# Channel-major filter and U for the first transform, with separate places for x

## What is computed

```python
h_filt = (np.maximum(pos_emb @ w1, 0) @ w2) * np.exp(-0.01 * pos)[:, None]   # 12480 x 128
u = x * v                                                                    # 12480 x 128
y = irfft(rfft(u, n=2*S) * rfft(h_filt, n=2*S))[:S]                          # per channel
a = x * y
a = np.maximum(a @ w_in, 0)**2 @ w_out                                       # 128 -> 2048 -> 128
h = a @ w_in2
out = (h / (1 + np.exp(-1.702 * h))) @ w_out2
```

## Time and profile before

| | |
|---|---|
| median of three runs | 1559.16 us |
| profiled execution | 1559.6 us |
| its span, first to last instruction | 1557.8 us |
| PE busy | 98% of the span |
| granted TensorE clock, mean | 0.998 |
| filter stage | 0 to 62.5 us |
| first transform, first half and second half | 62.5 to 117.5 and 246 to 299 us |
| inverse of the first half | 166.6 to 243 us |
| perceptrons | from 430 us |

### The profile page before, as it was taken

The page is one execution under the profiler, slowest core; times in us unless marked ns, Lnnn a source line. Parts: engine busy times, 40 slices in busy tenths (PEclk is TensorE's granted clock), DMA queues, the critical chain, the costliest instruction groups (busy, mean ns, idle before and its releaser), DMA issues.

```text
span 1557.8 us, 22645 instructions
## 1 busy us (share of the span) xinstructions
PE 1532.8 (98%) x7860; PEld 1458.2 (94%) x7860; DVE 992.7 (64%) x1315; ACT 943.0 (61%) x1217; POOL 270.0 (17%) x313
## 2 busy tenths in 40 slices
PE   7999999999989999999999999999999999999998
PEld 5898889988779999999999999999999999999997
DVE  4867686676656666666666666666666666666664
ACT  3353003431067777777777777777777777777775
POOL 5706791177710000000000000000000000000000
PEclk9999999999999999999999999999999999999999
DMA  7454720743000000000000000000000000000000
GB/s 179 110 83 126 138 41 26 115 113 105 1 0 1 7 10 5 5 5 5 5 5 5 5 5 5 5 5 5 5 5 5 5 5 6 10 5 5 5 7 11
DMA packets 93769, 46.89 MB, mean 30 GB/s; under 512 B 77705, under 2 KB 89337, under 8 KB 93481
## 3 DMA queue, kind: packets, MB, share of 16 engines
q1 hardware_dynamic: 92670, 45.80, 13.2%
q10 hardware_dynamic: 1067, 0.66, 0.1%
HBM read 40.06 MB, written 6.39 MB: 30 GB/s over the span
## 4 chain that ended last, share of the span: by engine, by line
PE 95%; DVE 3%; ACT 1%; issue 1%; DMA 0%; SPq 0%; ACTq 0%; DVEq 0%
PE ps L965 23%; PE ps L967 23%; PE ps L966 23%; PE ps L685 7%; PE ps L737 7%; PE ps L718 6%; PE ps L746 3%; DVE big L561 1%; PE ps L959 1%; PE ps L659 1%; PE ps L673 1%; PE ps L953 1%; PE ps L664 1%; DVE act_lo L940 0%; ACT act_f L890 0%
## 5 line engine op out<-in xcount | busy, mean ns | idle before, releaser
L940 DVE TENSOR_TENSOR act_lo<-act_f,act_hi 128x832 fp32r<-128x832 f32 x480 | 487.0, 1025 | 129.8 <-ACT act_hi L895 121.6
L965 PE MATMUL ps<-act_hi,w_hi 128*128 128x416 f32 x960 | 344.0, 358 | 1.3 <-DVE act_lo L940 1.3
L965 PE MATMUL ps<-in_hi,w_hi 128*128 128x416 f32 x960 | 337.8, 352 | 5.7 <-DVE in_lo L911 3.9
L967 PE MATMUL ps<-act_hi,w_lo 128*128 128x416 f32 x960 | 338.3, 352 | 0.0
L966 PE MATMUL ps<-in_lo,w_hi 128*128 128x416 f32 x960 | 336.0, 350 | 0.0
L966 PE MATMUL ps<-act_lo,w_hi 128*128 128x416 f32 x960 | 335.5, 349 | 0.0
L967 PE MATMUL ps<-in_hi,w_lo 128*128 128x416 f32 x960 | 334.1, 348 | 0.0
L938 DVE CAST act_hi<-act_f 128x832 fp32r<-128x832 f32 x240 | 148.4, 618 | 288.4 <-ACT act_f L890 288.4
L885 ACT ACTIVATE relu<-ps 128x832 f32<-128x832 f32 x240 | 208.3, 868 | 142.7 <-PE ps L967 138.8
L892 ACT ACTIVATE act_f<-ps 128x832 f32<-128x832 f32 x240 | 207.0, 863 | 117.7 <-PE ps L967 117.6
L890 ACT ACTIVATE act_f<-relu 128x832 f32<-128x832 f32 x240 | 216.0, 900 | 22.2 <-DVE act_lo L940 0.3
(11 more groups left out here) (64 smaller groups left out, 1401.2 us busy)
## 6 DMA issues: line engine op xcount, KB each, us to landing
f_ring<-in_fwd SPq DMA_DIRECT2D x52, 240.0 KB, 2.6
u_buf<-in_x SPq DMA_DIRECT2D x20, 312.0 KB
big<-in_v SPq DMA_DIRECT2D x20, 312.0 KB
filter_then_xy<-in_x SPq DMA_DIRECT2D x8, 780.0 KB
out<-rows SPq DMA_DIRECT2D x30, 208.0 KB
big<-in_pos_emb SPq DMA_DIRECT2D x40, 78.0 KB
u_buf<-in_moe_w_in SPq DMA_DIRECT2D x2, 1024.0 KB, 7.5
t<-in_inv ACTq DMA_DIRECT2D x1, 168.8 KB
```

The source lines that it names most:

```text
L940: nc.vector.tensor_tensor(lo[:, :, :], f[:, :, :], hi[:, :, :].bitcast(F32), ALU.subtract)\
L965: nc.tensor.matmul(to, w_hi[w][:, cols], hi, start=first, stop=False)
L967: return nc.tensor.matmul(to, w_lo[w][:, cols], hi, start=False, stop=last)
```

## The change

H and U become channel-major: `H[p, c, b]` and `U[p, c, b]`, with the 124 rows of a channel adjacent. The stationary operand of L685 is one contiguous run. The folds that write H and U read their operands through `by_channel`, rows innermost: the taps with a step of 128 elements, the U pieces with one of 64, and write runs of 3 rows (H) or 12 rows (U). `XY` is the same memory as H in its old order, for x and for x * y.

x of a piece cannot lie in U any longer. It gets slots of its own: five in the first half (three in `big` behind V, one in Y, one in `f_ring`), three in the second. SP therefore waits for the last U product before it loads the first four tables into `f_ring` in the first half, and in the second half it waits before pieces 3 and 4 until POOL has used the slot. The zero rows of U are set a second time in the first half, once all of P is made, since the spectra now overwrite some of them.

```diff
--- before.py
+++ after.py
@@ -150,7 +150,7 @@
     }
 
 
-def convolution(nc, block, sem, ALU, ACT, ds, F32, H, ps, u_buf, buf, weights, first_tile,
+def convolution(nc, block, sem, ALU, ACT, ds, F32, XY, ps, u_buf, buf, weights, first_tile,
                 x_d, v_d, pe_d, w1, w2, fwd1, fwd2_d, inv3, twiddle, inv4, window, identity):
 
 
@@ -177,7 +177,14 @@
     tw_prod = f_ring[0:A].rearrange("p s f g -> p (s f g)")\
         .rearrange("p (s t c r b) -> p s t c r b", s=2, t=2, c=2, r=2)
 
+    H = XY[:, :, :, :].rearrange("p h b c -> p (h b c)").rearrange("p (c b) -> p c b", b=BR)
+
     V = [carve(big, A, at, B, HC)[0] for at in (ZF, 0)]
+    x_slots = [[carve(big, A, at + B * HC + n * 2 * PB * HC, 2 * PB, HC)[0] for n in range(3)] for at in (ZF, 0)]
+    x_slots[0].append(Y[:, :, :, :, :].rearrange("p s r c b -> p (s r c b)")[:, 0:2 * PB * HC]
+                      .rearrange("p (b c) -> p b c", c=HC))
+    x_slots[0].append(f_ring[0:A].rearrange("p s f g -> p (s f g)")[:, 0:2 * PB * HC]
+                      .rearrange("p (b c) -> p b c", c=HC))
 
     pe_ring, at = carve(big, A, 0, RING, CB, FO)
     peT, at = carve(big, 128, at, RING, HB * A)
@@ -189,7 +196,7 @@
     ident, at = carve(big, 128, at, 128)
     taps, at = carve(big, A, at, RING, CB, D)
 
-    U, at = carve(u_buf, A, 0, BR, HC)
+    U, at = carve(u_buf, A, 0, HC, BR)
     t1, _ = carve(u_buf, A, at, 2 * A)
     h_spec, at = carve(u_buf, B, 0, 2, FG, 2, HC)
     prod_s, at = carve(u_buf, B, at, 2, FG, 2, HC)
@@ -266,13 +273,9 @@
         copy(to[ODD:BR, :, 0, c4].rearrange("p f (k c) -> p f k c", k=2), out[ODD:BR, :, :, :, 1])
         return negate(to[ODD:BR, :, 1, c4].rearrange("p f (k c) -> p f k c", k=2), out[ODD:BR, :, :, :, 0])
 
-    def h_rows(start, end):
-
-        return H[:, :, start:end, :].rearrange("p h b c -> p b h c")
-
-    def by_half(rows):
-
-        return rows.rearrange("p b (h c) -> p b h c", h=2)
+    def by_channel(rows):
+
+        return rows.rearrange("p b c -> p c b")
 
     def piece_rows(i):
 
@@ -283,9 +286,13 @@
         low, high, _ = piece_rows(i)
         return V[h][:, low], V[h][:, high]
 
+    def x_piece(h, i):
+
+        both = x_slots[h][i % len(x_slots[h])]
+        return both[:, 0:PB], both[:, PB:2 * PB]
+
     def load_x_piece(h, i):
-        low, high, high_rows = piece_rows(i)
-        for rows, to in ((low, U[:, low]), (high, U[:, high_rows])):
+        for rows, to in zip(piece_rows(i), x_piece(h, i)):
             nc.sync.dma_start(to, x_d[:, rows, h * HC:(h + 1) * HC]).then_inc(ld_u[i], 16)
 
     def load_v_piece(h, i):
@@ -365,7 +372,7 @@
                 sp.wait_ge(full[q], used["s1", h][q] + N1 // 2 // RING)
             for b in range(0, B, B // X_LOADS):
                 rows = slice(b, b + B // X_LOADS)
-                sp.dma_start(H[:, h, rows, :], x_d[:, rows, h * HC:(h + 1) * HC]).then_inc(ld_x, 16)
+                sp.dma_start(XY[:, h, rows, :], x_d[:, rows, h * HC:(h + 1) * HC]).then_inc(ld_x, 16)
 
         for i in range(ROUNDS):
             for s in range(RING):
@@ -376,7 +383,10 @@
         load_x_piece(0, PIECES - 1)
         load_v_piece(0, PIECES - 1)
         for h in range(2):
-            if h == 1:
+            if h == 0:
+
+                sp.wait_ge(u_made, 2 * PIECES)
+            else:
 
                 sp.wait_ge(y_made, 2 * N3)
             for s in range(RING):
@@ -393,6 +403,9 @@
             if h == 0:
 
                 for i in range(PIECES):
+                    if i >= len(x_slots[1]):
+
+                        sp.wait_ge(u_made, 2 * (PIECES + i - len(x_slots[1]) + 1))
                     load_x_piece(1, i)
                     load_v_piece(1, i)
             else:
@@ -409,10 +422,9 @@
     def _(pool):
         def make_u_half(h, i, high):
 
-            rows = piece_rows(i)
             pool.wait_ge(ld_u[i], 4 * 16 * (h + 1))
             v = v_piece(h, i)[high]
-            nc.gpsimd.tensor_tensor(v, v, U[:, rows[2 if high else 0], :], ALU.mult).then_inc(u_made, 1)
+            nc.gpsimd.tensor_tensor(v, v, x_piece(h, i)[high], ALU.mult).then_inc(u_made, 1)
 
         def make_u(h, i):
             make_u_half(h, i, 0)
@@ -426,15 +438,15 @@
                                     w_hi[m][:, cols].bitcast(F32), ALU.subtract).then_inc(w_split[m], 1)
 
         nc.gpsimd.memset(big[0:128, w_at:w_at + 2 * FO + 2 * D], 0.0).then_inc(bd_zero, 1)
-        nc.gpsimd.memset(H[:, :, B // 2:ODD, :], 0.0)
-        nc.gpsimd.memset(U[:, B // 2:ODD, :], 0.0)
+        nc.gpsimd.memset(H[:, :, B // 2:ODD], 0.0)
+        nc.gpsimd.memset(U[:, :, B // 2:ODD], 0.0)
         for i in range(ROUNDS):
             for s in range(RING):
                 n = i * RING + s
 
                 pool.wait_ge(free[s], i + 1)
-                nc.gpsimd.tensor_tensor(h_rows(BR - (n + 1) * HB, BR - n * HB), by_half(taps[:, s, 0:HB])[:, ::-1],
-                                        by_half(taps[:, s, HB:CB]), ALU.subtract).then_inc(h_odd[s], 1)
+                nc.gpsimd.tensor_tensor(H[:, :, BR - (n + 1) * HB:BR - n * HB], by_channel(taps[:, s, 0:HB])[:, :, ::-1],
+                                        by_channel(taps[:, s, HB:CB]), ALU.subtract).then_inc(h_odd[s], 1)
             if i > 0:
                 make_u(0, i - 1)
         make_u(0, PIECES - 1)
@@ -450,6 +462,11 @@
             for s in range(NG % RING - 1):
                 combine(F_FULL, s)
 
+            if h == 0:
+
+                for b in range(2):
+                    pool.wait_ge(p_done[b], P_USES[b])
+                nc.gpsimd.memset(U[:, :, B // 2:ODD], 0.0)
             U_AT = {2 + 2 * i + high: (i, high) for i in range(PIECES) for high in range(2)}
             SPLIT_AT = {2 + 2 * m * SPLITS + 2 * part: (m, part) for m in range(3) for part in range(SPLITS)}
             for k in range(N3):
@@ -541,10 +558,11 @@
             low, _, high_rows = piece_rows(i)
             u_low, u_high = v_piece(h, i)
             if odd:
-                made = nc.vector.tensor_tensor(U[:, high_rows, :], u_low[:, ::-1], u_high, ALU.subtract)
+                made = nc.vector.tensor_tensor(U[:, :, high_rows], by_channel(u_low)[:, :, ::-1], by_channel(u_high),
+                                               ALU.subtract)
             else:
                 dve.wait_ge(u_made, 2 * (h * PIECES + i + 1))
-                made = nc.vector.tensor_tensor(U[:, low, :], u_low, u_high[:, ::-1], ALU.add)
+                made = nc.vector.tensor_tensor(U[:, :, low], by_channel(u_low), by_channel(u_high)[:, :, ::-1], ALU.add)
             made.then_inc(u_folded, 1)
 
         def fold_u(h, i):
@@ -562,8 +580,8 @@
                     taps[:, s], flat[s][0:A, 0:CB * D].rearrange("p (b c) -> p b c", b=CB),
                     win[:, n * CB:(n + 1) * CB].unsqueeze(2).to_broadcast([A, CB, D]), ALU.mult).then_inc(free[s], 1)
                 dve.wait_ge(free[s], i + 1)
-                nc.vector.tensor_tensor(h_rows(n * HB, (n + 1) * HB), by_half(taps[:, s, 0:HB]),
-                                        by_half(taps[:, s, HB:CB])[:, ::-1], ALU.add).then_inc(h_even[s], 1)
+                nc.vector.tensor_tensor(H[:, :, n * HB:(n + 1) * HB], by_channel(taps[:, s, 0:HB]),
+                                        by_channel(taps[:, s, HB:CB])[:, :, ::-1], ALU.add).then_inc(h_even[s], 1)
             if i > 1:
                 fold_u(0, i - 2)
         for h in range(2):
@@ -613,13 +631,13 @@
 
             def multiply_x(k):
                 q, count = inv_slot(4, k, h)
-                xy = H[:, h, 0:B, 4 * k:4 * k + 4]
+                xy = XY[:, h, 0:B, 4 * k:4 * k + 4]
                 dve.wait_ge(full[q], count)
                 nc.vector.tensor_tensor(
                     xy, slot[q][0:A, 0, 0:4 * B].rearrange("p (c b) -> p b c", c=4), xy, ALU.mult).then_inc(free[q], 1)
 
             def stage_channels(half, start, end):
-                return nc.vector.tensor_copy(stage[:, :, half * HC + start:half * HC + end], H[:, half, 0:TB, start:end])
+                return nc.vector.tensor_copy(stage[:, :, half * HC + start:half * HC + end], XY[:, half, 0:TB, start:end])
 
             dve.wait_ge(ld_x, 16 * X_LOADS * (h + 1))
             FOLD_U_AT = {4 + 2 * i + odd: (i, odd) for i in range(PIECES) for odd in range(2)}
@@ -680,7 +698,7 @@
             pe.wait_ge(free[q], used["s1", h][q] + k // RING)
             for e in range(4):
                 c = (4 * k + e) % HC
-                data = H[:, h, :, c] if k < N1 // 2 else U[:, :, c]
+                data = H[:, h * HC + c, :] if k < N1 // 2 else U[:, c, :]
                 at = e % 2 * 2 * A
                 mm = nc.tensor.matmul(slot[q][0:BR, e // 2, at:at + 2 * A], data, t1[:, :],
                                       start=True, stop=True)
```

## The result

Ten runs of the changed kernel have a median of 1563.28 us (1558.53 to 1567.17), ten of the kernel before 1559.37 us (1558.67 to 1560.35). The ratio is 1.0021, with a 95% interval of 1.0013 to 1.0030: slower by 2.0 to 4.7 us by the interval, by 3.9 us in the medians. The profiled execution took 1563.81 us, with a span of 1562.0 against 1557.8.

What follows compares the result with a forecast made beforehand. The first transform, PE alone in both halves, was taken as bound by its strided stationary loads. Terms -15.0 + 13.3 + 2 + 2.5 + 1.5 = +4.3 gave 1563.5 us at the median, range 1543 to 1582.

Steps and rivals of the forecast that it cites:

- turning point: Filter stage: the forecast sum is zero where a chunk on POOL costs about 1.9 us instead of 1.43.
- Gain of the transform: L685, both halves: contiguous stationary loads take a record from 213.3 to 184 ns, 15.0 us less (12.4 to 19.1).
- Price of the hop: Folds on DVE and POOL: hopping operands multiply the part that grows with the elements by 1.62.
- Start: First transform, first half: slower filter folds on POOL delay its beginning from 62.55 to about 75.9 us, +13.3 us.
- Clock: Beginning of the first transform, after PE's idle time: lower granted clock costs half of 4 us, +2 us.
- Stalls: First transform: U folds of pieces 3 and 4 delay PSUM copies; PE waits 0.6 and 1.2, 2.5 us in all.
- Inverse: First half's inverse: longer U folds make POOL lag 3.8 us against a lead of 2.8, +1.5 us (0 to 6).
- Edits costed at nothing: x slots, later table and piece loads, second memset and row order through XY: claimed to cost 0 us.
- A: Folds of H and U: striding costs nothing on DVE and POOL; 1544 us (1540 to 1547), chance 0.17.
- B: Folds of H and U: DVE pays for striding, POOL's own part doesn't; 1554 us, chance 0.17.
- C: Filter stage: POOL pays about twice, a chunk takes over about 2.8 us; 1583 us, chance 0.16.
- D: First transform: the stationary load isn't what holds PE, 213 ns a record stay; 1578 us, chance 0.05.

Runs made afterwards that it cites:

- the version without stalls: The changed kernel with taps written channel-major by the window product and U folds in groups of 2 rows; 1541.06 us, ratio 0.9884.
- the spare products: The changed kernel with ten more filler products on PE ahead of its wait for the odd folds; 1560.88 us, ratio 1.0008.

## Why the prediction was right, and where it was not

The total (1563.5 forecast, 1563.28 measured), the sign and the mechanism came as forecast: the vector engines pay for PE's new layout, POOL's unbroken chain delays the first transform, PE's hole costs clock, the U folds ahead of groups 5 and 9 stall PE and lengthen the first inverse. That the total fell within 0.2 us is luck. The gain was 3.2 us larger than forecast and the start 2.5 us less late, while clock, stalls and inverse cost 5.4 more. The forecast's own turning point shows it: a chunk of 1.9 us on POOL was to mean no change. The chunk came at 1.88, and the kernel is 3.9 us slower.

- **Gain of the transform**, 15.0 us forecast. The second half gives -9.0, and the version without stalls has 55.7 - 46.45 = 9.2 in the first: 18.2. The pace is 175.9 ns and not 184, the bound set by the moving operand. The step that failed is the reading of the perceptrons' 189 ns as their stationary load: 124 contiguous columns follow each other in 176 ns, so 183 was no bound for them; what sets the 189 is not known.
- **Price of the hop**, one ratio of 1.62 for all. It fitted POOL's own part (1.38 measured, 1.39 forecast), but not DVE: the filter fold hardly pays (0.60 against 0.80 forecast), the U fold pays double (1.9 against 1.43). The ratio from PE's loads was a stand-in and has nothing to say on the inner length.
- **Start**, +13.3 forecast, +10.8 measured: a chunk has a pace of 1.88 and not 2.17, since DVE's share of it hardly grew. That alone would be 4.6 us less; the U folds, longer than forecast, took part of it back.
- **Clock**: +2 forecast behind the hole, 1.9 measured with the spare products. The second fall, behind group 9, another 1.7 us (0.26 and 0.17 of two windows of 4 us), was not in the sum.
- **Stalls** ahead of groups 9 and 13: 0.6 and 1.2 forecast, 2.5 with POOL's wait; the holes are 1.12 and 2.16, 3.3 in all. The place was right. The form, two folds and three copies against three groups, isn't exact: with 1.9 for 1.43 it gives 1.5 and 3.1.
- **Inverse**, +1.5 forecast, +4.5 measured. Beside POOL the fold grew by 0.64 and not by 0.48 (1.43 to 2.07), though alone it grew by 1.0. At step 11 POOL ends 65.9 us after the stage's start and not 60.4: 5.5 of lag where 3.8 were forecast. Less the lead of 2.8, PE has lost 2.8 there, and 1.7 more in the steps behind it, for which the forecast had 0.5.
- **Edits costed at nothing**: the run with x slots only shows them at 0.
- **Rivals.** A falls with POOL's 1.88 and the U folds' 1.9; B has DVE and POOL exchanged, in the filter stage POOL pays and DVE doesn't; C's price isn't reached, the chunk takes 1.88 us where C begins at about 2.8; D falls with 175.9 ns.

The rule of the Trainium skill quoted in the prediction (Vector Engine (DVE) Microarchitecture Reference, the SBUF access granule) holds for the U folds with 4 rows and more, which pay more than its 1.75 ns (1.9 us less 0.17 over 768 elements is 2.3 ns an element). It doesn't hold for inner runs of 2 and 3 rows: both sources hop at every element and the fold takes 1.05 to 1.15 ns an element. There the measurement decides. The 50% that the Trainium skill gives for wide read steps (GPSIMD Engine Reference, performance pitfalls, stated there for kernels on its Q7 cores) agrees with POOL's fold here, 0.89 to 1.38.

## What to carry to other kernels

A layout is paid by whoever makes the transposition: before a buffer is turned for one engine's reads, look up who writes it, whether that engine is on the chain, and do the turn where the hop is free, here in DVE's read of PSUM. Where an operand must hop in SBUF, try the order of the loops inside the same instruction, since here 3 rows inside instead of 12 decided between a loss and a gain. And two engines that exclude each other share one budget: a longer operation on one is waited for by the other, and a short hole of PE behind it can be paid again in clock.

## What was not expected of the hardware

- DVE, two SBUF sources with a step of 64 elements: 768 elements in 0.98 us with 2 rows inside, 1.05 with 3, 1.7 to 1.8 with 4 and 1.85 with 6 (these two in one run), 1.9 with 12, against 0.95 contiguous. The length of the written runs changed with it.
- POOL pays for hopping reads (0.89 to 1.38 us for 384 elements) and not for hopping writes (about 0.8, in one run); DVE pays for writes that hop (0.56 to 0.86, in the same run).
- TensorE, stationary operand of 124 columns: with a step of 64 elements a record takes 213 ns, contiguous 176.
- DVE reads PSUM with a step of 128 elements as fast as in order (768 elements in 0.95 us).
- 124 contiguous stationary columns keep up with a moving operand of 208 float32 columns: 175.9 ns a record, as much as 104 columns.
